# Two expert stages behind a gated attention: GpSimd's splits and sums in another order, and finer waits

## The reference

```python
# attention, per head: state[d, e] = alpha[t, d] * state[d, e] + k[t, d] * v[t, e];  y[t, e] = sum_d q[t, d] * state[d, e]
# 2 batches, 8 heads, 768 steps, 48 wide; y becomes x: 1536 tokens x 384
rms = np.sqrt(np.mean(x * x, axis=-1, keepdims=True) + 1e-06)
xn = x / rms * rms_g
g = xn @ w_gate                      # 384 x 1536
silu = g * (1.0 / (1.0 + np.exp(-g)))
x = (silu * (xn @ w_val)) @ w_out    # 1536 x 384
p = domain_probs / (domain_probs.sum(-1, keepdims=True) + 1e-09)
for e in range(4):                   # w1: 4 x 384 x 1024, w2: 4 x 1024 x 384
    out += p[:, e:e + 1] * (np.maximum(x @ w1[e], 0.0) @ w2[e])
```

## Time and profile before

| | |
|---|---|
| time, median of 3 runs | 716.4 us (716.32 to 719.37) |
| time of the profiled execution | 716.6 us |
| its span, first to last instruction | 714.9 us |
| TensorE busy | 692.0 us (97%), 3996 matmul records |
| VectorE, ScalarE, GpSimd busy | 462.3 us (65%), 262.2 us (37%), 319.5 us (45%) |
| mean granted TensorE clock | 0.99 |
| chain that ended last | PE 85%, POOL 3%, SPq 3%, issue 3%, DMA 2%, DVE 2%, ACT 1% |
| DMA | 35.13 MB, mean 49 GB/s |

### The profile page before, as it was taken

One profiled execution on the slowest core, in us unless ns is written; L12 is line 12 of the kernel. 1 busy time (PEld: TensorE's weight loads), 2 busy tenths in 40 slices (PEclk: granted clock), 3 DMA queues, 4 the chain that ended last, 5 costly groups with the idle time before them and its releaser, 6 DMA issues.

```text
span 714.9 us, 10681 instructions
## 1 busy us (share of the span) xinstructions
PE 692.0 (97%) x3996; PEld 639.8 (89%) x3996; DVE 462.3 (65%) x802; ACT 262.2 (37%) x477; POOL 319.5 (45%) x402
## 2 busy tenths in 40 slices
PE   6879999999999999899989999999999999999998
PEld 5669999999999999799889999999999999999997
DVE  5774666565555633614956778777876778777876
ACT  3831225222432243124513344333443344343430
POOL 3457671111111113931076755576556755576200
PEclk8899999999999999999999999999999999999999
DMA  8994461003202000200001011100111011100003
GB/s 180 201 194 106 103 133 34 1 9 79 56 1 75 1 1 19 71 1 1 0 23 46 1 44 45 45 29 16 45 45 44 1 46 44 45 23 1 22 1 133
DMA packets 71748, 35.13 MB, mean 49 GB/s; under 512 B 53904, under 2 KB 70672, under 8 KB 71696
## 3 DMA queue, kind: packets, MB, share of 16 engines
q1 hardware_dynamic: 71696, 34.44, 19.4%
HBM read 31.48 MB, written 2.36 MB: 47 GB/s over the span
## 4 chain that ended last, share of the span: by engine, by line
PE 85%; POOL 3%; SPq 3%; issue 3%; DMA 2%; DVE 2%; ACT 1%; DVEq 0%; POOLq 0%
PE out_ps L1304 13%; PE out_ps L1306 12%; PE out_ps L1305 12%; PE hid_ps L1297 7%; PE hid_ps L1299 6%; PE hid_ps L1298 6%; PE at_ps L1488 4%; PE at_ps L1487 4%; PE at_ps L1486 4%; SPq L451 2%; PE hid_ps L1487 2%; PE hid_ps L1488 2%; PE hid_ps L1486 2%; PE at_ps L1342 2%; PE at_ps L1356 1%
## 5 line engine op out<-in xcount | busy, mean ns | idle before, releaser
L1182 DVE SCALAR_TENSOR_TENSOR x<-out_ps,prob,x 128x384 f32<-128x384 f32 x180 | 110.3, 613 | 58.6 <-PE out_ps L1306 58.6
L1304 PE MATMUL out_ps<-early_r,late_r 128*128 128x384 f32 x384 | 129.1, 336 | 0.6 <-DVE x L1182 0.5
L1305 PE MATMUL out_ps<-early_r,late_r 128*128 128x384 f32 x384 | 129.4, 337 | 0.0
L1306 PE MATMUL out_ps<-early_r,late_r 128*128 128x384 f32 x384 | 129.3, 337 | 0.0
L670 POOL TENSOR_TENSOR hid_lo<-act_sb,hid_hi 128x384 fp32r<-128x384 f32 x44 | 44.9, 1021 | 179.2 <-ACT hid_hi L854 179.2
L895 ACT COPY late<-at_ps 128x512 f32<-128x512 f32 x98 | 57.7, 589 | 110.4 <-PE at_ps L1488 107.6
L1147 DVE TENSOR_TENSOR act_sb<-hid_ps,act_sb 128x384 f32<-128x384 f32 x48 | 26.6, 555 | 80.3 <-PE hid_ps L1299 71.1
L1304 PEld LDWEIGHTS out_ps<-early_r,late_r 128*128 128x128 f32 x384 | 72.1, 188 | 6.8 <-DVE x L1182 1.0
L1305 PEld LDWEIGHTS out_ps<-early_r,late_r 128*128 128x128 f32 x384 | 72.0, 188 | 5.3
L1306 PEld LDWEIGHTS out_ps<-early_r,late_r 128*128 128x128 f32 x384 | 72.1, 188 | 0.0
L723 POOL TENSOR_TENSOR early<-stage 128x128 f32<-128x128 f32 x14 | 6.6, 471 | 132.5 <-PE at_ps L1488 101.4
(11 more groups left out here) (256 smaller groups left out, 1622.5 us busy)
## 6 DMA issues: line engine op xcount, KB each, us to landing
stage<-in_moe_w_dram SPq DMA_DIRECT2D x32, 384.0 KB, 3.6
alpha_all<-in_alpha_dram SPq DMA_DIRECT2D x8, 288.0 KB, 5.9
stage<-in_moe_w_out_dram SPq DMA_DIRECT2D x4, 576.0 KB, 3.9
out_dram<-x SPq DMA_DIRECT2D x12, 192.0 KB, 1.9
stage<-in_moe_w_gate_dram SPq DMA_DIRECT2D x8, 216.0 KB, 3.9
stage<-in_moe_w_val_dram SPq DMA_DIRECT2D x8, 216.0 KB, 4.2
a_tm<-in_alpha_dram SPq DMA_DIRECT2D x9, 192.0 KB, 3.3
k_tm<-in_k_dram SPq DMA_DIRECT2D x9, 192.0 KB, 3.9
```

The source lines that it names most:

```text
L1182: dve.scalar_tensor_tensor(out=a, in0=part, scalar=p, in1=a, op0=ALU.mult, op1=ALU.add).then_inc(s_acc, 1)
L1304: pe.matmul(dst, ah, bh, start=first, stop=False)
L1305: pe.matmul(dst, ah, bl, start=False, stop=False)
L1306: return pe.matmul(dst, al, bh, start=False, stop=last)
```

## The change

It has seven edits.

1. `EARLY` is 3 in place of 4: GpSimd splits three pieces ahead of its loop, and in it one piece behind each `hidden_lo` of passes 0 to 8 (before: 0 to 7). SyncE's order of loads is as it was.
2. In the last quarter, `plain_weights` and `out_weights` of the first two pairs stand one by one behind `hidden_lo` of passes 0, 1, 2 and 3; before, both of a pair stood behind passes 0 and 1.
3. `first_sums` stands behind passes 4, 5 and 6, not 2, 3, 4 and 5.
4. ScalarE rounds two or three token sums behind each of the first five banks of plain products; before, one behind each of eleven.
5. VectorE's last two `split_sum` stand ahead of the third bank of pair 1, and its first `add_up` ahead of the last bank's lower half.
6. TensorE's wait for the token blocks' lower halves in `hidden_plain` is for one block before each three matmuls, not for three blocks before the first.
7. In the last pair only, `add_up` of tile 9 stands one instruction earlier on VectorE.

```diff
-        EARLY = 4
+        EARLY = 3
...
-            for n in range(EARLY + 1, NPIECE):
+            for n in range(5, NPIECE):
...
-            if n == EARLY - 1:
+            if n == EARLY:
                 pool.wait_ge(s_xl, KT)
...
             def first_sums(f):
-                if f == 2:
+                if f == 4:
...
-                elif f == 3:
+                elif f == 5:
...
-                elif f == 4:
+                elif f == 6:
...
-                elif f == 5:
...
-                    if i == NQ - 1:
+                    if i == NQ - 1 and f > 3:
                         first_sums(f)
                     if i == 0 and f < NPIECE - EARLY:
                         split(pool, EARLY + f)
-                    if i == NQ - 1 and f < PLAIN:
+                    if i == NQ - 1 and f < 2 * PLAIN:
                         if f == 0:
                             pool.wait_ge(s_xl, KT * NQ)
-                        plain_weights(f)
-                        out_weights(f)
+                        if f % 2:
+                            out_weights(f // 2)
+                        else:
+                            plain_weights(f // 2)
...
-            for pair in range(PLAIN):
-                for n in range(6):
-                    act.wait_ge(s_plain, 6 * pair + n + 1)
-                    round_hidden(sums[n], pair, n % 2, n // 2)
-                    k = 6 * pair + n
-                    if k < len(V_DONE):
-                        round_sum(V_DONE[k])
+            def round_plain(pair, n):
+                act.wait_ge(s_plain, 6 * pair + n + 1)
+                round_hidden(sums[n], pair, n % 2, n // 2)
+
+            round_plain(0, 0)
+            for k in range(2):
+                round_sum(V_DONE[k])
+            round_plain(0, 1)
+            for k in range(2, 5):
+                round_sum(V_DONE[k])
...
+            round_plain(0, 5)
+            for n in range(6):
+                round_plain(1, n)
...
             split_sum(8)
-            split_plain(1, 2)
             split_sum(9)
             split_sum(10)
-            split_plain(1, 3)
-            split_plain(1, 4)
+            for n in range(2, 5):
+                split_plain(1, n)
+            dve.wait_ge(s_xbh, len(BLOCKS))
+            add_up(0, 0)
             split_plain(1, 5)
-            dve.wait_ge(s_xbh, len(BLOCKS))
-            for t in range(NTILE):
+            for t in range(1, NTILE):
                 add_up(0, t)
...
                 combine(bank_b, 6, ALU.subtract)
+                if pair == NPAIR - 1:
+                    add_up(pair - 1, 9)
                 dve.wait_ge(s_add, nth(ADDS, q, 8))
                 combine(bank_d, 5, ALU.add)
-                add_up(pair - 1, 9)
+                if pair < NPAIR - 1:
+                    add_up(pair - 1, 9)
...
-                    if pair == 0:
-                        pe.wait_ge(s_xbl, KT * (t + 1))
...
-                        product(sums[n], [((wph[pair][:, j, cols], wpl[pair][:, j, cols]), (xh[j, t], xl[j, t]))
-                                          for j in range(KT)]).then_inc(s_plain, 1)
+                        for j in range(KT):
+                            if pair == 0 and f == 0:
+                                pe.wait_ge(s_xbl, KT * t + j + 1)
+                            mm = accumulate(sums[n], (wph[pair][:, j, cols], wpl[pair][:, j, cols]),
+                                            (xh[j, t], xl[j, t]), j == 0, j == KT - 1)
+                        mm.then_inc(s_plain, 1)
```

More of the change, by code:

```diff
@@ L885, in _ @@
             act.wait_ge(s_o, FT * NQ)
-            for pair in range(PLAIN):
-                for n in range(6):
-                    act.wait_ge(s_plain, 6 * pair + n + 1)
-                    round_hidden(sums[n], pair, n % 2, n // 2)
-                    k = 6 * pair + n
-                    if k < len(V_DONE):
-                        round_sum(V_DONE[k])
+            def round_plain(pair, n):
[7 more added lines that the diff above has]
+                round_sum(V_DONE[k])
+            round_plain(0, 2)
+            round_sum(V_DONE[5])
+            round_sum(V_DONE[6])
+            round_plain(0, 3)
+            round_sum(V_DONE[7])
+            round_sum(V_DONE[8])
+            round_plain(0, 4)
+            round_sum(V_DONE[9])
+            round_sum(V_DONE[10])
+            round_plain(0, 5)
+            for n in range(6):
+                round_plain(1, n)
             def keep(n, bank):
```

## The result

The changed kernel takes 706.1 us (median of 4 runs, 705.57 to 706.63) where the kernel before took 716.4 beside it (714.57 to 719.37, 4 runs). The ratio is 0.985, with a 95% interval of 0.982 to 0.989. The forecast was 705.8. The profiled execution took 705.96 us, its span 704.2 us, 10.7 us less than before.

What follows compares the result with a forecast made beforehand. TensorE was taken as the bound, so only its waits could give time back: 4.6 + 3.3 + 2.7 + 0 = 10.6 us off 716.6 gave 706.0, or 705.8 from the median of 716.4; range 703.9 to 709.5 us.

Steps and rivals of the forecast that it cites:

- part 1: Three early pieces in place of four, near 50 us: gain 4.6 us, bounds 2.7 and 5.0.
- part 1: wait and restart: TensorE's first output product starts at 50.3 us, not 53.60: 3.3 us won plus 0.1 for the restart.
- part 1: clock: Without the idle stretch, no half-rate clock from 54.13 to 57.54 us: 1.6 us won, low end 0.
- part 1: new wait at value product 2: Pass 2's value product waits for pass 1's upper product on VectorE: 0.3 us lost plus 0.1 for the restart.
- part 2: Last quarter, second stage's weight splits over four passes: TensorE's waits at 287 and 294 us go, 3.3 us; bounds 0, 3.4.
- part 3: Seam from first to second expert stage: waits at 335.85, 362.81 and 372.44 us shrink, 2.7 us; bounds 0.5 and 2.9.
- part 4: Last pair, tile at 697.76 us starts 0.6 earlier but VectorE is full: counted 0, bounds -0.1 and 0.5.
- Rival (d): GpSimd, 55 to 100 us: later splits starve TensorE of first-stage weights, 15.6 us lost, 720.8 us; chance 0.03.
- Rival (b): Clock still falls near 54 us or the new wait is longer: part 1 gives 2.7, 707.7 us; chance 0.10.
- the scaling: VectorE's twelve probability-tile scalings behind pass 2's product, last quarter: 8.93 us before, forecast done near 292.7 us.
- a fourth tile's wait: Seam: with the third tile earlier, the fourth may wait 0.15 us.
- third tile's gain: Seam, 362.81 us: VectorE's first accumulation moved ahead of the last bank's lower half starts the tile 0.26 + 0.10 us earlier.

Runs made afterwards that it cites:

- the filler: Kernel before with 12 small fp32 constant products in TensorE's idle stretch ahead of its first output product: 714.8 us against 716.2, ratio 0.998.
- the first repeat: The kernel before, run once more unchanged to see whether the clock falls in each run: 714.4 us.
- early-sums experiment: Changed kernel with GpSimd's seven token sums begun in pass 2 of the last quarter again, the weights left spread: 708.9 us.

## Why the prediction was right

The time was 0.3 us off, and the large terms were found where they were forecast. That the sum meets so closely is in part luck: a loss that was not forecast (0.49) went against a start-up that came 0.26 us earlier and a new wait that was 0.2 shorter. The terms, forecast and found:

| term | forecast | found (leads) |
|---|---|---|
| part 1: wait and restart | 3.4 | 3.31 |
| part 1: clock | 1.6 | 1.54 |
| part 1: new wait at value product 2 | -0.4 | -0.22 |
| part 2 | 3.3 | 3.4 |
| part 3: three places | 2.2, 0.3, 0.35 - 0.15 | 2.17, 0.34, 0.34 |
| part 4 | 0 | 0.07 |
| not forecast: squares of the second quarter, with drifts | none | -0.49 |
| start-up of this run | none | 0.26 |
| sum | 10.6 | 10.7 |

**Part 1** held step by step. The lower half began at 47.44 (47.7 forecast), TensorE at 50.03 (50.3), both earlier by the start-up's 0.26 us, the new wait came where it was expected, and the splits of pieces 4 and later hid in GpSimd's idle time. Rival (d) had no footing: all of GpSimd's waits for first-stage weight DMAs lie before 38 us. Its time was also summed wrongly: 705.8 + 15.6 is 721.4 us, not 720.8. The clock term was right for the execution that was profiled, but right for a reason I had not stated: the fall is not a property of the program. Over many runs that term is worth less than 1.5 us, about three fifths of it by the traces; the filler's 1.7 (0.6 to 2.7) allows either. The median before, 716.0 to 716.4 in each set of runs, happened to lie beside a profile with one fall: here the prediction was lucky. The forecast time hangs on it less than the gain does, since a profile without the fall is shorter by what the term would have promised: from the first repeat's 714.4 us, 10.6 less 1.6 gives an estimate of 705.4 us. Rival (b) gave the clock term to chance in the wrong place: it asked whether the changed kernel would still lose its clock, and should have asked how often before did. Part 3 holds such a chance too, which the sum left out: the wait that it removed at the seam had a fall behind it in 2 of 7 traces.

**Part 2** came out as forecast, and the step behind it was the one that mattered: GpSimd runs dry behind one block, and the scaling ends in the gap. The forecast had the twelve in 5 to 6 us and pass 3's product 0.8 us ahead of TensorE; they took 4.76, and the product ended at 288.72, 1.0 us ahead of 289.71. The three long ones of the estimate were there (1035, 887 and 1836 ns), and the nine short ones started 0.13 us apart; the 0.14 of the forecast stands in none of its rows. The early-sums experiment agrees with that margin: a scaling 2.27 us longer, less 1.0, makes 1.3 us, and TensorE lost 1.44. The Trainium skill, "SBUF — State Buffer", section "Who interferes with whom", says that such a VectorE instruction and a GpSimd one exclude each other for the whole instruction. The traces agree: 1840 ns beside GpSimd's 1.93 us, 217 to 220 ns with GpSimd idle. But not all of the twelve are caught. Behind each of GpSimd's L656 and L664 that met the twelve, one or two short ones slipped through before its next instruction, behind the others none. So the twelve cost about as much as the GpSimd instructions that they meet, not twelve of them.

**Part 3** held: the first weight sum came 3.8 us earlier against TensorE's work (348.67 + the lead of 8.1 there = 356.8, against 360.57 before), where 4 was forecast. The 0.15 us of a fourth tile's wait did not come. The third tile's gain I gave to the moved accumulation alone, and it needs ScalarE's order. The finer wait and VectorE's own new order at the seam were not undone by themselves, so their shares are read from the leads and not shown by a run.

**Part 4** held: VectorE's sum of work is the same, and the wait moved by 2.3 us.

**What was missed** is the start at 107.94. I had checked that the later splits were in time for their users, but not what they now run beside. In before, GpSimd had finished the last piece at 106.51, 4 us before VectorE added the squares:

```profile
110.79 0.56 DVE L1095 TENSOR_TENSOR x_nrm<-x_nrm 128x384 f32<-128x384 f32 x1 [2.47 <-ACT x_nrm L770]
```

Now its last subtraction (105.85 to 106.88) lies on the addition, which reads twice from SBUF and took 1.27 us in place of 0.56. The same section of the Trainium skill's "SBUF — State Buffer" states this case too: a VectorE instruction with two SBUF inputs contends with a GpSimd instruction that reads SBUF. I had used its other rule, for the scaling, and not carried this one to the moved splits. It cost 0.37 us at that start, and the experiment that holds the subtraction back brings the same 0.37 back.

## What to carry to other kernels

When instructions of GpSimd move, ask three things, not one: who waits for them, what they now wait for, and which VectorE instructions they now lie beside. Then set the matmuls of both traces side by side, start against start: the difference dates each gain and each loss to a tenth of a microsecond, where the medians of four runs differ by a whole one from start-up and clock alone. And a stretch at half clock in one profile is one draw of several: before its microseconds go into a sum, look at a second profile of the same program.

## What the runs showed of the hardware

- The granted clock fell to 0.50 behind a TensorE wait of 2 to 4 us in 5 of 12 such places and in none of the 14 where the wait was filled or missing, each time for 1.2 to 1.6 us of delay; the same program did it at 54 us in one run and not in another. The Trainium skill, "TensorE: Matmul & The Clock Gate", section "What's actually happening", says that the number of slow matmuls at the start of one kernel varies from run to run. The traces show that of the falls in the middle of a kernel as well.
- A small fp32 product of 128 columns is two records and 0.22 to 0.24 us (24 of them 5.5 us, 12 of them 2.84), not one of 0.12.
- Twelve VectorE instructions of 4 elements took 2.5, 4.8, 6.7, 7.0 or 8.9 us; what changed between these runs was what GpSimd did beside them.
